# Products of 128 columns that nobody reads, in TensorE's waits at the start of a fused attention and expert kernel

## The chip, the cores and the metric

The kernel runs on one core of a Trainium2 chip. The metric is the device time of one execution in microseconds (us), as the median of several executions. The traced execution has a time of its own. Engines are named as the profile names them: PE is TensorE (matrix products and transposes), PEld is its weight load, DVE is VectorE, ACT is ScalarE, POOL is GpSimd, SP is the engine that issues most transfers.

## The reference

Three stages follow one another. First comes attention over 2 batches, 8 heads, 576 rows and 64 columns a head, in which each row of scores keeps only its 32 largest values:

```python
scores = scale * np.matmul(q, k.transpose(0, 1, 3, 2))
kth = np.partition(scores, -top_k, axis=-1)[..., -top_k:-top_k + 1]
scores = np.where(scores >= kth, scores, -1000000000.0)
attn = exp(scores - max) / sum
x = np.matmul(attn, v)
```

Then a top-1 mixture of 8 experts (512 to 1024 to 512 columns, 288 slots an expert), and last a dense layer (512 to 2048 to 512) with a rational function between its two products.

## The kernel before

**Tiling.** The 1152 rows of queries (both batches) are cut into 9 tiles of 128. A step of the attention is one tile and one head, so there are NH = 72 steps. `slot(i)` is what an engine does around step i; every engine has such a function, and all of them run through the same steps at different distances.

**What PE does in the attention.** Keys and queries are held as a high and a low part. `k_turn(g, half)` (line 1354) turns half a head of keys with six or three transposes of 96 columns and waits for the low part of that head, which DVE makes for heads 0 and 1 (line 766) and POOL for the others (line 605), out of what ACT made of the rows loaded (`k_high`, line 1110). `q_turn` (line 1367) turns four heads of queries, once for the high part and once for the low. ACT takes what was turned out of PSUM (`k_out`, line 1080, `q_out`, line 1101), but for the first high part of the queries, which DVE takes (line 775). `scores(x)` (lines 1389 and 1390) makes the 576 scores of a row in four products of 288 columns. It waits until keys and queries are turned and taken, and until DVE's first instruction on the scores before (`greater`, line 784) has freed the two banks `S_ps`. `turn_scores`, `less_max` and `drop` (lines 1401, 1411, 1418) turn the scores of step i - 2 into the other pair of banks, `T_ps`; nothing else is written there, and the first of them starts with slot 2. `times_v` (line 1435) multiplies by the values, from slot 3.

**What the others do.** ACT copies the scores to SBUF (`scores_out`, line 1123), POOL sums and subtracts the two halves of a row (lines 629 and 636), and DVE finds the 32 largest: line 784 once a step, then eight-wide maxima (lines 801 and 822) and replacements (lines 803 and 820). The smallest value kept goes to ACT for `short_of` (line 1131).

**The order at the start.** Each engine runs its program in order. PE's is: both halves of key head 0, queries high and low (heads 0 to 3), key head 1, `scores(0)`, `scores(1)`, key head 2, queries high and low (heads 4 to 7), key head 3, a wait for POOL's fill of the values' column of ones (`s_vo`, line 687), and then slots 0 to 71, where slot i begins with `scores(i + 2)` and slots 0 to 3 turn key heads 4 to 7. ACT's is: `k_high(0)`, `q_high(0)`, `k_high(1)`, `k_out` of head 0, `q_out` low, `k_out` of head 1, `k_high(2)`, `scores_out(0)`, `k_high(3)`, `scores_out(1)`, `k_out` of head 2, `q_out` high and low, `k_high(4)`, `k_out` of head 3, and then its slots, the first of which begins with `scores_out(2)`. Keys come in three transfers: heads 0 and 1, heads 2 to 7, and the second batch.

**The function used by the change.** `keep_busy` (line 1442) exists already; the kernel calls it between the experts and the dense layer with 512 columns:

```python
def keep_busy(times, to, by):
    for _ in range(times):
        nc.tensor.matmul(to, by[:, 0:P], by[:, 0:to.shape[1]], start=True, stop=True)
```

It signals nothing. `ones` is a constant of 128 by 128 that POOL writes first of all (line 594, after which `s_const` is 1).

Of the kernel before, what the change touches and what calls it, by code (L numbers as in the profile page):

```python
# [22 lines left out]
P = 128  # L23
# [5 lines left out]
NH = NT * H  # L29
# [28 lines left out]
def fused(nc, q, k, v, w_gate, w1, w2, w_in, w_out, a, b, out):  # L58

    ctx = ExitStack()  # L60
    with ctx:
# [5 lines left out]
        def sem(name):  # L67
            return ctx.enter_context(nc.semaphore(name))
# [81 lines left out]
        def small(name, shape, dt=F32):  # L150
            nonlocal o
            n = 2 if dt == BF16 else 4
            for d in shape[1:]:
                n *= d
            t = at(name, o, shape, dt)
            o += -(-n // 32) * 32
            assert base + o <= nc.sbuf_usable_end
            return t
        ident = small("ident", [P, P])
        tri = small("tri", [P, P], F32R)  # L160
        ones = small("ones", [P, P], F32R)
# [27 lines left out]
        T_ps = pb[1]  # L189
# [19 lines left out]
        s_const = sem("constants")  # L209
# [123 lines left out]
        def is_mixed(n):  # L333
            return n == MIXED

        def batches(n):
            return range(B) if is_mixed(n) else [n // (TPB + 1)]
# [6 lines left out]
        def k_pieces(i):  # L344

            n, h = divmod(i, H)
            if n == 0:
                return [(FIRST_K + h, half) for half in range(2)] if FIRST_K + h < H else []
            if n in (1, 2):
                return [(H + (n - 1) * (H // 2) + h // 2, h % 2)]  # L350
            return []
# [5 lines left out]
        def q_pieces(i):  # L357

            n, h = divmod(i, H)
            if h == 0:  # L360
                return [(n, 1, 1)] if 0 < n < NT else []
            if n >= LAST:
                return []
            return {3: [(n + 1, 0, 0)], 4: [(n + 1, 1, 0)], 7: [(n + 1, 0, 1)]}.get(h, [])

        def x_piece(i):

            n, h = divmod(i, H)
            return n - 1 if h == 6 and 0 < n < NT else None

        def logit_piece(i):

            n, h = divmod(i, H)
            if i == NH - 1:
                return LAST - 1
            return n - 2 if h == 0 and 1 < n < NT else None
# [27 lines left out]
        def emptied(use):  # L404

            assert use != BY_DVE
            return use + 1 - (use > BY_DVE)
# [928 lines left out]
        def _(pe):  # L1336
# [8 lines left out]
            def k_turn(g, half):  # L1345
                use = USE["k", g, half]
                if g < 2:
                    pe.wait_ge(s_kl[0], g + 1)
                else:
                    pe.wait_ge(s_kl[1], g - 1)  # L1350
                prep_in(use)
                for c in range(KJ // 2):
                    j = half * (KJ // 2) + c
                    last = nc.tensor.transpose(prep_bank(use)[:, c * KP:(c + 1) * KP],
                                               ks[g % KRING][:, j].rearrange("k t d -> k (t d)").bitcast(F32),
                                               ident[0:KP, 0:KP])
                last.then_inc(s_pf, 1)
# [12 lines left out]
            def scores(x):  # L1370

                n, h = divmod(x, H)
                if x == 0:
                    pe.wait_ge(s_pd, 1)
                pe.wait_ge(s_pe, max(emptied(USE["q", n, 1, h // (H // 2)]),
                                     max(emptied(USE["k", bb * H + h, 1]) for bb in batches(n))))
                if x:
                    pe.wait_ge(s_gr, x)
                for half in range(2):
                    dst = S_ps[:, half * BANK:half * BANK + HS]  # L1380
                    off = h * S + half * HS
                    if is_mixed(n):
                        for bb in range(B):
                            for low in range(2):
                                last = nc.tensor.matmul(dst, qTm[:, low, bb, h, :], kT[bb][:, off:off + HS],
                                                        start=(bb + low == 0), stop=(bb + low == 2))
                    else:
                        keys = kT[batches(n)[0]][:, off:off + HS]
                        nc.tensor.matmul(dst, qTh[:, h, :], keys, start=True, stop=False)
                        last = nc.tensor.matmul(dst, qTl[:, h, :], keys, start=False, stop=True)  # L1390
                last.then_inc(s_qk, 1)

            def turn_scores(x):

                pe.wait_ge(s_sc, x + 1)
                if x == NH - 1:
                    pe.wait_ge(s_gr, NH)
                elif x:
                    pe.wait_ge(s_ex, x)
                for j in range(KJ):  # L1400
                    nc.tensor.matmul(turned(x)[0:KP, j * P:(j + 1) * P], sc[x % NS][:, j * KP:(j + 1) * KP], ident[:],  # L1401
                                     start=(j in (0, 4)), stop=False, is_transpose=True, skip_group_check=True)

            def less_max(x):

                pe.wait_ge(s_mh, 2 * x + 2)
                for lo, hi in ((0, 4), (4, KJ)):
                    dst = turned(x)[0:KP, lo * P:hi * P].rearrange("k (j q) -> k j q", q=P)
                    each = minus_one[:].unsqueeze(1).to_broadcast([P, hi - lo, P])
                    for part in (mh, ml):  # L1410
                        nc.tensor.matmul(dst, part[x % 2][:].to_broadcast([P, KP]), each, start=False, stop=False,  # L1411
                                         skip_group_check=True)

            def drop(x):

                pe.wait_ge(s_so, x + 1)
                for j in range(KJ):
                    last = nc.tensor.matmul(turned(x)[0:KP, j * P:(j + 1) * P], so[x % 2][:, j * KP:(j + 1) * KP], minus_big[:],  # L1418
                                            start=False, stop=(j in (3, KJ - 1)), skip_group_check=True)
                last.then_inc(s_tt, 1)  # L1420

            def times_v(x):
                n, h = divmod(x, H)
                k_ = x // XG
                dst = bank(4 + k_ % 2)[:, (x % XG) * DV:(x % XG + 1) * DV]
                pe.wait_ge(s_ex, x + 1)
                if x < 2 * XG:
                    pe.wait_ge(s_pe, emptied(FIRST - 1))
                elif x % XG == 0:
                    pe.wait_ge(s_xe, k_ - 1)  # L1430
                for bb in batches(n):
                    pe.wait_ge(*((s_v[2], 16 * H) if bb else (s_v[1], 16 * (H - 2)) if h >= 2 else (s_v[0], 32)))
                    r_ = slice(bb * HALF, (bb + 1) * HALF) if is_mixed(n) else slice(0, P)
                    for j in range(KJ):
                        last = nc.tensor.matmul(dst[r_, :], pT[x % 2][:, j * P + r_.start:j * P + r_.stop],  # L1435
                                                vn[:, bb * H + h, j, :], start=(j == 0), stop=(j == KJ - 1))
                last.then_inc(s_pv, 1)
# [5 lines that stand above are left out]
# [57 lines left out]
                    last.then_inc(s_fx, 1)  # L1500

            def slot(i):
                if i + 2 < NH:
                    scores(i + 2)
                if 0 <= i - 3 < NH:
                    times_v(i - 3)
                if 0 <= i - 2 < NH:
                    turn_scores(i - 2)
                    less_max(i - 2)
                    drop(i - 2)  # L1510
                for k_ in k_pieces(i):
                    k_turn(*k_)
                for q_ in q_pieces(i):
                    q_turn(*q_)
                if x_piece(i) is not None:
                    turn_x(x_piece(i))
                if logit_piece(i) is not None:
                    logits(logit_piece(i))

            pe.wait_ge(s_ident, 3)  # L1520
            k_turn(0, 0)
            k_turn(0, 1)
# [2 lines left out]
            k_turn(1, 0)  # L1525
            k_turn(1, 1)
            scores(0)
            scores(1)
            k_turn(2, 0)
            k_turn(2, 1)  # L1530
# [3 lines left out]
            k_turn(3, 1)  # L1534
            pe.wait_ge(s_vo, 1)
            for i in range(NH):
                slot(i)
            for x in (NH - 2, NH - 1):
                turn_scores(x)
                less_max(x)  # L1540
                drop(x)
# [159 lines left out]
```

## Time and profile before

| what | value |
|---|---|
| time, median of 3 executions | 792.28 us (792.05 to 793.22) |
| time of the profiled execution | 790.87 us |
| its span, first to last instruction | 789.1 us |
| mean granted TensorE clock | 0.988 |
| PE busy | 750.9 us (95%), 5482 products |
| DVE busy | 664.5 us (84%) |
| ACT busy | 496.7 us (63%) |
| POOL busy | 368.5 us (47%) |

The span is the profiler's and leaves out 1.77 us that the execution's own time has around it. Busy times are sums over stages with different limits, so the share of an engine alone doesn't tell what sets the end. A product's duration includes its way through the array and overlaps with the next one, so the distance between two starts tells what a product costs. In a line of a timeline several alike are merged: the duration is then that of all of them.

### The profile page before, as it was taken

How to read it: one execution, taken by the hardware profiler on the slowest of the kernel's cores; microseconds unless marked ns; L12 is line 12 of the kernel's file. 1: busy time of each engine (PE TensorE's matmuls, PEld its weight loads, DVE VectorE, ACT ScalarE, POOL GpSimd, SP SyncE). 2: the span in 40 equal slices, each digit the busy share in tenths (PEclk: the TensorE clock that was granted, in tenths of full speed). 3: DMA queues.
4: the chain of work that ended last, by engine and by line, in shares of the span. 5: the costliest groups of instructions: out<-in, count | busy, mean ns of one | idle time of the engine just before them, and what ended most of it. 6: DMA issues, size and time to landing. Idle time of an engine off the chain costs nothing.

```text
span 789.1 us, 15796 instructions
## 1 busy us (share of the span) xinstructions
PE 750.9 (95%) x5482; PEld 700.7 (89%) x5482; DVE 664.5 (84%) x1677; ACT 496.7 (63%) x898; POOL 368.5 (47%) x540
## 2 busy tenths in 40 slices
PE   5899999999999999899999999999899999999997
PEld 4788899898888888789999999999779898998996
DVE  3999999999999999986666766675759998888885
ACT  6677777566677776474444444444547877677674
POOL 3746665554558785362000000000059778666764
PEclk8899999999999999999999999999999999999999
DMA  8640000800000203015475768686810002001001
GB/s 184 155 184 14 1 16 1 225 8 13 15 2 15 108 2 108 2 43 216 137 243 168 230 180 256 175 208 185 238 54 27 1 1 81 1 0 41 1 1 40
DMA packets 60811, 70.63 MB, mean 90 GB/s; under 512 B 21953, under 2 KB 40769, under 8 KB 60738
## 3 DMA queue, kind: packets, MB, share of 16 engines
q1 hardware_dynamic: 59298, 64.98, 28.6%
q0 software_dynamic: 1440, 4.72, 1.8%
q8 instruction: 41, 0.67, 0.4%
q14 instruction: 32, 0.26, 0.1%
HBM read 55.53 MB, written 14.16 MB: 88 GB/s over the span
## 4 chain that ended last, share of the span: by engine, by line
PE 58%; DVE 27%; DMA 5%; issue 5%; ACT 2%; POOL 2%; SPq 1%; DVEq 0%; ACTq 0%; POOLq 0%
PE bank L1564 16%; PE bank L1566 15%; PE bank L1565 15%; DVE best L801 9%; DVE pairs L803 6%; PE bank L1435 3%; DVE best L822 3%; DVE pairs L784 3%; DVE pairs L820 3%; DMA slots_out<-y_blocks 2%; PE bank L1411 2%; PE bank L1401 2%; DMA slot_rows<-slots_in 1%; DMA k_rows<-in_k 1%; DVE joined L831 1%
## 5 line engine op out<-in xcount | busy, mean ns | idle before, releaser
L1066 DVE RECIPROCAL r<-c 128x384 f32<-128x384 f32 x48 | 122.4, 2551 | 20.6 <-POOL c L740 19.7
L801 DVE MAX8 best<-pairs 128x8 f32<-128x288 f32 x288 | 116.8, 450 | 0.0
L1137 ACT ACTIVATE probsT<-bank 96x768 f32<-96x768 f32 x72 | 58.1, 807 | 90.8 <-PE bank L1418 88.4
L729 POOL DMA_INDIRECT x_rows<-slots_out,slot_index x9 | 10.5, 1165 | 210.2 <-DMA slots_out<-y_blocks 208.6
L1435 PE MATMUL bank<-v_rows,probsT 96*128 96x65 f32 (+1 forms) x960 | 105.8, 263 | 2.6 <-ACT probsT L1137 2.5
L1435 PEld LDWEIGHTS bank<-v_rows,probsT 96*128 96x128 f32 (+1 forms) x960 | 101.9, 181 | 6.8 <-ACT probsT L1137 5.6
L989 DVE TENSOR_TENSOR wl<-raw,wh 128x1024 fp32r<-128x1024 f32 x72 | 87.2, 1218 | 19.0 <-ACT wh L1245 18.9
L803 DVE MATCH_REPLACE8 pairs<-best,pairs 128x288 f32<-128x288 f32 x216 | 95.7, 450 | 0.0
L1262 ACT ACTIVATE hTh<-bank 128x288 fp32r<-128x288 f32 x64 | 26.4, 413 | 102.5 <-PE bank L1566 102.5
L629 POOL TENSOR_TENSOR pairs<-scores 128x288 int32<-128x288 int32 x72 | 57.5, 799 | 66.3 <-ACT scores L1123 66.0
L1245 ACT ACTIVATE wh<-raw 128x1024 fp32r<-128x1024 f32 x72 | 75.1, 1051 | 4.1 <-DMA raw<-in_moe_w_out 3.2
L1564 PE MATMUL bank<-xTh,wh 128*128 128x288 f32 x256 | 75.7, 296 | 1.0 <-DVE xTl L1006 0.7
L1564 PE MATMUL bank<-hTh,wh 128*128 128x288 f32 x256 | 75.7, 296 | 0.6 <-DVE hTl L1027 0.6
L1566 PE MATMUL bank<-hTh,wl 128*128 128x288 f32 x256 | 76.1, 297 | 0.0
L1565 PE MATMUL bank<-hTl,wh 128*128 128x288 f32 x256 | 75.8, 296 | 0.0
L1565 PE MATMUL bank<-xTl,wh 128*128 128x288 f32 x256 | 75.6, 295 | 0.0
L1566 PE MATMUL bank<-xTh,wl 128*128 128x288 f32 x256 | 75.1, 293 | 0.0
L740 POOL TENSOR_TENSOR c<-c,h 128x384 f32<-128x384 f32 x48 | 48.6, 1013 | 48.4 <-ACT h L1323 48.3
L1564 PE MATMUL bank<-x2h,wh 128*128 128x384 f32 x192 | 65.8, 343 | 0.5 <-DVE g L1073 0.3
L822 DVE MAX8 best<-pairs 128x8 f32<-128x288 f32 x144 | 66.1, 459 | 0.0
L1566 PE MATMUL bank<-x2h,wl 128*128 128x384 f32 x192 | 64.7, 337 | 0.0
L1565 PE MATMUL bank<-x2l,wh 128*128 128x384 f32 x192 | 64.4, 336 | 0.0
(160 smaller groups left out, 2195.5 us busy)
## 6 DMA issues: line engine op xcount, KB each, us to landing
raw<-in_moe_w SPq DMA_DIRECT2D x15, 2048.0 KB, 8.9
slots_in<-zeros SPq DMA_DIRECT2D x18, 256.0 KB
slots_out<-y_blocks SPq DMA_DIRECT2D x32, 144.0 KB, 8.1
raw<-in_moe_w_in SPq DMA_DIRECT2D x8, 512.0 KB, 8.0
slot_rows<-slots_in SPq DMA_DIRECT2D x28, 144.0 KB, 9.0
v_rows<-in_v SPq DMA_DIRECT2D x16, 144.0 KB, 4.2
out_rows<-out_rows SPq DMA_DIRECT2D x9, 256.0 KB, 2.4
q_rows<-in_q SPq DMA_DIRECT2D x8, 256.0 KB, 3.3
```

The costliest lines, as they stand in the source:

```text
L629: nc.gpsimd.tensor_tensor(pr[x % NPR][:, 1].bitcast(I32), of[:, 0:HS], of[:, HS:S], ALU.add).then_inc(s_ps, 1)
L801: ins = nc.vector.max(best, cur)
L803: ins = nc.vector.match_replace(cur, best, cur, NEG)
L822: ins = nc.vector.max(best, cur)
L989: nc.vector.tensor_tensor(piece(wl[slot], c), piece(raw[which], c), piece(wh[slot], c).bitcast(F32), ALU.subtract).then_inc(s_wl, 1)
L1066: nc.vector.reciprocal(rS[x][:], cS[x][:]).then_inc(s_d2, 1)
L1137: nc.scalar.activation(pT[x % 2][:], turned(x)[0:KP, 0:KJ * P], ACT.Exp, scale=SCALE).then_inc(s_ex, 1)
L1245: nc.scalar.activation(piece(wh[slot], c), piece(raw[which], c), ACT.Copy).then_inc(s_wh, 1)
L1435: last = nc.tensor.matmul(dst[r_, :], pT[x % 2][:, j * P + r_.start:j * P + r_.stop], vn[:, bb * H + h, j, :], start=(j == 0), stop=(j == ...
L1564: nc.tensor.matmul(dst, ah, bh, start=start, stop=False)
L1565: nc.tensor.matmul(dst, ah, bl, start=False, stop=False)
L1566: return nc.tensor.matmul(dst, al, bh, start=False, stop=stop)
```

## The change

Ahead of the first transposes PE waits for `ones` and multiplies `ones` by itself 40 times into the first 128 columns of `T_ps`. After `scores(0)` it does so 24 times. `scores(2)` and `scores(3)` are issued ahead of slots 0 and 1 rather than as their first piece (in the same place of PE's order), and after them stand 12 and 8 such products, and behind slots 0 and 1 another 6 and 14: 104 in all. The order of what was there stays, and nothing is changed on the other engines.

```diff
             def slot(i):
-                if i + 2 < NH:
+                if 2 <= i < NH - 2:
                     scores(i + 2)
...
+            pe.wait_ge(s_const, 1)
+            keep_busy(40, T_ps[:, 0:P], ones)
             pe.wait_ge(s_ident, 3)
             k_turn(0, 0)
...
             scores(0)
+            keep_busy(24, T_ps[:, 0:P], ones)
             scores(1)
...
             for i in range(NH):
+                if i < 2:
+                    scores(i + 2)
+                    keep_busy((12, 8)[i], T_ps[:, 0:P], ones)
                 slot(i)
+                if i < 2:
+                    keep_busy((6, 14)[i], T_ps[:, 0:P], ones)
```

## Rows read from the trace of the kernel before

**Rows 1.** Page, the span in 40 slices of 19.7 us: busy tenths and granted clock.

```profile
PE   5899999999999999899999999999899999999997
...
DVE  3999999999999999986666766675759998888885
...
PEclk8899999999999999999999999999999999999999
```

**Rows 2.** Stretches: length; busy us and (instructions) per engine; clock, DMA share, GB/s.

```profile
240.00:280.00 40.00, 37.16 (x322) 34.34 (x321) 40.00 (x157) 30.22 (x51) 31.42 (x52) 1.00 0.18 61
```

**Rows 3.** Timeline of VectorE: start us, us, what, count, [idle before it <- releaser].

```profile
14.94 0.46 DVE L784 TENSOR_TENSOR pairs<-bank,scores 128x288 f32<-128x288 f32 x1 [2.16 <-ACT scores L1123]
...
16.64 0.09 DVE L803 MATCH_VALUE_LOAD pairs<-best,pairs 128x8 f32 x1 [0.87 <-POOL pairs L636]
...
18.66 0.45 DVE L822 MAX8 best<-pairs 128x8 f32<-128x288 f32 x1
...
20.19 0.46 DVE L784 TENSOR_TENSOR pairs<-bank,scores 128x288 f32<-128x288 f32 x1 [1.09 <-ACT scores L1123]
...
24.79 0.44 DVE L784 TENSOR_TENSOR pairs<-bank,scores 128x288 f32<-128x288 f32 x1
```

**Rows 4.** Timeline of ScalarE, from 8 to 20 us.

```profile
8.27 1.19 ACT L1101 ACTIVATE qT_low<-bank 64x512 fp32r<-64x512 f32 x2 [1.29 <-PE bank L1367]
...
11.23 0.52 ACT L1110 ACTIVATE k_split<-k_rows 96x384 fp32r<-96x384 f32 x1 [1.04 <-DMA k_rows<-in_k]
...
14.26 0.65 ACT L1123 ACTIVATE scores<-bank 128x576 f32<-128x576 f32 x1 [1.56 <-PE bank L1390]
...
16.07 1.19 ACT L1101 ACTIVATE qT_high<-bank 64x512 fp32r<-64x512 f32 x2 [0.44 <-PE bank L1367]
...
18.51 0.52 ACT L1110 ACTIVATE k_split<-k_rows 96x384 fp32r<-96x384 f32 x1
...
19.52 0.64 ACT L1123 ACTIVATE scores<-bank 128x576 f32<-128x576 f32 x1
```

**Rows 5.** Timeline of TensorE's products, from 5 to 21 us.

```profile
5.33 1.19 PE L1354 MATMUL bank<-ident,k_split 96*128 96x96 f32 x6 [5.33 <-DVE k_split L766]
...
8.02 0.84 PE L1354 MATMUL bank<-ident,k_split 96*128 96x96 f32 x6
...
9.60 0.37 PE L1389 MATMUL bank<-kT,qT_high 128*128 128x288 f32 x1 [0.74 <-ACT qT_low L1101]
...
10.08 0.29 PE L1390 MATMUL bank<-kT,qT_low 128*128 128x288 f32 x1
...
12.93 0.58 PE L1389 MATMUL bank<-kT,qT_high 128*128 128x288 f32 x1 [2.56 <-DVE pairs L784]
...
13.78 0.44 PE L1390 MATMUL bank<-kT,qT_low 128*128 128x288 f32 x1
...
20.16 0.72 PE L1354 MATMUL bank<-ident,k_split 96*128 96x96 f32 x6 [1.34 <-POOL k_split L605]
```

**Rows 6.** Stretches of 1 us in which the granted clock changes; the column before DMA share.

```profile
11.00:12.00 1.00, 0.00 (x0) 0.00 (x0) 0.00 (x0) 0.77 (x2) 0.16 (x1) 0.90 0.81 153
...
18.00:19.00 1.00, 0.82 (x4) 0.51 (x3) 1.00 (x4) 0.97 (x3) 0.00 (x0) 0.69 1.10 244
...
22.00:23.00 1.00, 0.57 (x4) 0.57 (x5) 1.00 (x5) 1.00 (x3) 1.00 (x2) 0.52 1.15 188
```

**Rows 7.** Timeline of TensorE's products: eight short ones and what follows, full clock.

```profile
345.57 1.03 PE L1459 MATMUL bank<-wg,x_tileT 128*128 128x8 f32 x8 [0.17 <-issue]
...
346.46 0.77 PE L1495 MATMUL bank<-slot_of_token,x_high 128*128 128x288 f32 x4
```

**Rows 8.** Timeline of TensorE's weight loads at the lower clock.

```profile
17.49 0.33 PEld L1389 LDWEIGHTS bank<-kT,qT_high 128*128 128x128 f32 x1
...
17.70 0.33 PEld L1390 LDWEIGHTS bank<-kT,qT_low 128*128 128x128 f32 x1
```

**Rows 9.** Timeline of GpSimd: the constant that the new products read.

```profile
0.80 0.20 POOL L594 MEMSET ones<- 128x128 f32 x1 [0.29 <-POOLq L1690]
```

## The prediction

> **What bounds the kernel now.** I began with the page's slices. PE is busy at 9 tenths nearly everywhere, and the granted clock falls short in the first two slices alone, which is where the change works [rows 1]. DVE is at 9 in every slice from the third to the sixteenth. In a stretch of 40 us in the middle of the attention it is busy for all 40.00 us, PE for 37.16 [rows 2]. So the attention ends when DVE has done its list. A faster PE brings nothing there, unless it lets DVE begin its unbroken work earlier.
>
> Where does that begin? The timeline of DVE has its last long wait, 1.09 us for ACT's copy of the scores, ahead of the instruction at 20.19 [rows 3]. Whatever makes that copy earlier moves all that follows.
>
> So I followed ACT back [rows 4]. `scores_out(2)` at 19.52 comes behind a block without a pause that starts at 16.07. That block waited 0.44 us for PE's transposes of queries. The block before starts at 14.26, after 1.56 us of waiting for PE's `scores(1)`. Before that ACT waits for the second transfer of keys, which lands at 11.23: nothing that PE does can make that earlier.
>
> Last I read PE's clock. The windows show it fall to 0.50 within 11 to 12 us, rise in 18 to 19 and fall again at 22 [rows 6]. The value 1.00 at the very beginning is not to be believed: the six transposes take 1.19 us at 5.33, against 0.72 at 20.16, and 0.84 at 8.02 [rows 5]. So PE starts at the lower level, 1.2 GHz, and rises to 2.4 GHz near 8 us, some 2.7 us after its first product. `scores(0)` runs at full clock (9.60 to 10.08, 0.48 us from first to last start), `scores(1)` at half (12.93 to 13.78, 0.85 us) [rows 5]. In between PE waited 2.56 us for DVE, and the clock fell.
>
> **The price of one product.** None like it (128 columns, full weights) is in the trace. Eight products of 8 columns with weights as large take 0.89 us from 345.57 to 346.46 [rows 7], so 0.11 us each at full clock, a bound from weight loading. At half clock two loads start 0.21 us apart [rows 8]. Below, with streaming alone, it would be 0.85/3 x 128/288 = 0.126 us at half clock and 0.48/3 x 128/288 = 0.07 us at full [rows 5]. I take 0.11 and 0.21, since the loads are needed for each product; 0.07 and 0.126 are the lower ends.
>
> **40 ahead of the first transposes.** `ones` is written at 1.0 us [rows 9]; I start at 1.1. If the clock rises 2.7 us later as before, at 3.8, then 13 are done at 0.21 and 27 take 3.0 us: the end is at 6.8. If it rises only after 4.8 us, the end is at 7.2. The transposes were ready at 5.33 [rows 5], so PE starts them 1.5 to 1.9 us late. But they run at full clock by then. From 5.33 until ACT could take the low queries at 8.27 [rows 4] was 2.94 us; at twice the clock that is 1.5, so 8.3 to 8.7 instead of 8.27. ACT had 1.04 us to spare ahead of 11.23 [rows 4]. So this costs nothing; the cover ends if the first transposes start after 8.27 + 1.04 - 1.5 = 7.8 us.
>
> **24 after `scores(0)`.** The last of it starts at 10.08, so they run from about 10.2 (10.6 at the late end) for 24 x 0.11 = 2.64 us, to 12.8 (13.2). `scores(1)` began at 12.93 [rows 5]. Cost 0 to 0.3; I take 0.1 at most, since a later `scores(0)` is likely to be by less. What they buy: `scores(1)` at full clock. It is 0.37 us shorter from first to last start, and its last product shorter by 0.15 (0.44 against 0.29), so ACT's copy starts near 13.75 instead of 14.26: **0.5 us**.
>
> **Transposes between `scores(1)` and slot 0.** ACT got the queries' high part 1.81 us after it had got `scores(1)` (16.07 less 14.26), and had work for 1.37 of them [rows 4]. At twice the clock the 1.81 become 0.9, so the queries are there when ACT comes, and the 0.44 us of waiting go as well. ACT's list from 14.26 on then stands without a hole: 0.5 + 0.44 = 0.95 us earlier at `scores_out(2)`. `greater(2)` on DVE moves from 20.19 to 19.2 or 19.3. The next in line is DVE itself: its own last maximum of step 0, at 18.66 + 0.45 = 19.1 even if nothing before it moves [rows 3]. So not much more than 1.1 us can be had here.
>
> **12 after `scores(2)`, 6 after key head 4.** PE waited 1.34 us there for POOL's low keys [rows 5]; 12 x 0.11 = 1.3 fit in. The 6 put 0.66 us in front of `scores(3)`, which followed the transposes of 20.16 at once. It would come at 20.5 or so instead of 20.8. DVE wants `scores(3)` at 24.79 [rows 3], so it has more than 3 us in hand. Cost nothing.
>
> **8 after `scores(3)`, 14 after key head 5.** 22 x 0.11 = 2.4 us, between `scores(3)` (20.9 at the latest start before) and `scores(4)`, which cannot start before DVE's instruction of 24.79 [rows 3]: nearly 4 us, with one short transpose inside. Cost nothing. What they buy is that the clock doesn't fall at 22 us [rows 6]. `scores(4)` and the first turned scores run in half the time, but DVE had no hole after 20.19, so this is worth nothing at the end. No queue but PE's is passed: no transfer is added or moved, and nobody waits for the products.
>
> **Sum.** 0 for the 40, + 0 to 0.1 for the 24, - 0.5 and - 0.44 for ACT's list, 0 for the other 40 products: -0.95 us, between -0.85 and the -1.1 of DVE's own list. Against the profiled execution: 790.87 - 0.95 = 789.9. The runs' median is 1.41 above that execution; I carry the difference to it: 792.28 - 0.95 = 791.3 us. Everything after the attention follows in a chain, so the shift should last to the end. About 0.2% (1.6 us) is what a measurement can tell from none, and this is 0.12%.
>
> **The rivals.** (a) **The short products don't lift the clock** (slower). Half of a product's slot is weight loading, 0.11 against 0.05 of columns; in the trace the clock fell in spite of 1.4 us of work after 20.16 [rows 5, 6]. Then the 40 take 8.4 us and end at 9.5, later than the deciding point 7.8. The chain of 2.94 us at half clock follows, ACT gets the low queries at 12.4 instead of 8.27, 4.1 late less 1.04 of slack: +3.1. After `scores(0)` 24 x 0.21 = 5.0 us stand where PE waited 2.6: +2.4. Together +5.5, 797.8 us. At the lower end of 0.126 us the 40 end at 6.1 and are hidden, and the 24 cost 0.4: 792.7. Between the two ends, at 0.17, it is 1.1 + 6.8 + 2.94 - 8.27 - 1.04 = +1.5, and 4.1 - 2.6 = +1.5: 795.3. The likely half of it is 794.3 to 797.8. For it: no row shows the clock under such a mixture. Against: what was needed before 18.69 was no more than transposes and `scores(1)`.
>
> (b) **The transposes don't keep what the products won** (no change). The clock rises early but falls again over the transposes, and the 0.95 us are lost: 792.2. Against: the clock rose near 8 us when PE had done only transposes [rows 5], and in 18 to 19 us after mostly those [rows 6]. The Trainium skill ("TensorE: Matmul & The Clock Gate", Part 4) says that the full clock doesn't engage for transposes, since they don't count as busy in the same way; by that rule this rival would hold. The trace disagrees with it: 0.84 us for six transposes at 8.02 against 1.19 at 5.33.
>
> (c) **More than I see** (faster by 1.6 us and more): the runs stand 1.2 to 2.4 us above the profiled one, and if part of it is clock lost at the start, the products give that back too: 789.5 to 790.6. For it speaks only that difference.
>
> **How the numbers follow.** Forecast 0.55, (a) 0.20, (b) 0.12, (c) 0.13. Of the forecast a tenth or two reaches over 1.6 us by the measurement. Faster by over 0.2%: 0.13 + 0.10 = 0.23. Slower: 0.20, and 0.01 of mishaps. The rest, 0.56, within 0.2%. The range reaches down to 789.8, into (c), and up to 794.3, short of (a), which leaves out some 0.2 in all; the forecast's own range is 790.7 to 792.0.
>
> **What would show it.** Right: the first transposes start between 6.4 and 7.5 us with 0.72 us for six, products of line 1442 are 0.11 us apart, the clock reads 1.00 in every stretch up to 34 us, ACT's copy of `scores(1)` is at 13.7 and `greater(2)` at 19.2. The 24 end before DVE frees the banks. Wrong: products 0.21 us apart up to the end, transposes after 7.8 us, ACT's `k_high(2)` later than the transfer at 11.2, or a DVE wait that comes up after 20 us and takes the microsecond back.

## The result and the profile after

| | before | after |
|---|---|---|
| time, median | 791.90 us (788.66 to 793.22, 15 executions) | 797.61 us (794.36 to 801.88, 15 executions) |
| ratio | | 1.0085 (95% interval 1.0066 to 1.0105) |
| profiled execution, span | 790.87, 789.1 us | 797.61, 795.8 us |

The change made the kernel slower by 0.85%, and its executions spread wider. (The ratios in this document are estimates with an interval and not the quotient of the two medians, which is 1.0072 here. The two can differ by 0.1%, so effects of that size are read from traces.) I had forecast 791.3 us with a range of 789.8 to 794.3.

From the page of the changed kernel, its span and the slices that answer to [rows 1]:

```profile
span 795.8 us, 16004 instructions
...
PE   9999999999999999899999999999899999999997
...
DVE  1799999999999999986666667665759998888885
...
PEclk9999999999999999999999999999999999999999
```

The granted clock stands at 9 in all slices, where before it began with two eights. By this line the change did what it was for, and PE is full from the first slice. But DVE reads 1 and 7 where it read 3 and 9: it begins later. The 6.7 us that the span grew by all lie there. The last of DVE's searches (its smallest kept value of step 71) comes at 342.62 us, against 335.67 before, 6.95 later; `greater(2)`, the start of its unbroken work, comes 7.07 later.

PE's timeline of the changed kernel, as in [rows 5]:

```profile
1.06 8.80 PE L1442 MATMUL bank<-ones 128*128 128x128 f32 x40 [1.06 <-POOL ones L594]
...
9.65 1.18 PE L1354 MATMUL bank<-ident,k_split 96*128 96x96 f32 x6
...
13.91 0.58 PE L1389 MATMUL bank<-kT,qT_high 128*128 128x288 f32 x1 [0.41 <-ACT qT_low L1101]
...
14.77 0.45 PE L1390 MATMUL bank<-kT,qT_low 128*128 128x288 f32 x1
15.01 5.22 PE L1442 MATMUL bank<-ones 128*128 128x128 f32 x24
...
20.02 0.55 PE L1389 MATMUL bank<-kT,qT_high 128*128 128x288 f32 x1
...
25.25 0.41 PE L1389 MATMUL bank<-kT,qT_high 128*128 128x288 f32 x1
...
27.73 0.86 PE L1442 MATMUL bank<-ones 128*128 128x128 f32 x6
...
28.43 0.35 PE L1389 MATMUL bank<-kT,qT_high 128*128 128x288 f32 x1
```

The 40 products take from 1.06 to 9.65, **0.215 us each to the very end**, and the 24 take from 15.01 to 20.02, 0.209 us each. The clock doesn't rise in 8.6 us of unbroken products. `scores(0)` at 13.91 is slow as well (0.58 us for its first product; 0.37 at full clock, [rows 5]). It stays low to the last product of `scores(0)` (0.45 us at 14.77, 0.29 at full clock), so the transposes and `scores(0)` between 9.65 and 15.01 didn't lift it either in this execution. It rises near 25.3 us, when PE has done its transposes again and is in `scores(2)`; from there the same products take 0.12 us each (six from 27.73 to 28.43).

And this is how the window of 17 to 18 us reads in the middle of the 24 (columns as in [rows 2], the granted clock third from the end):

```profile
17.00:18.00 1.00, 1.00 (x7) 1.00 (x7) 0.00 (x0) 0.00 (x0) 0.73 (x1) 1.00 1.01 252
```

1.00, while every duration is at half clock. The record of the granted clock shows nothing before its first change. The clock line of the page was no witness here; the durations were.

ACT and DVE of the changed kernel, as in [rows 4] and [rows 3]:

```profile
12.58 1.19 ACT L1101 ACTIVATE qT_low<-bank 64x512 fp32r<-64x512 f32 x2 [1.30 <-PE bank L1367]
...
14.39 0.52 ACT L1110 ACTIVATE k_split<-k_rows 96x384 fp32r<-96x384 f32 x1
...
21.33 0.65 ACT L1123 ACTIVATE scores<-bank 128x576 f32<-128x576 f32 x1 [5.02 <-PE bank L1390]
```

```profile
15.93 0.46 DVE L784 TENSOR_TENSOR pairs<-bank,scores 128x288 f32<-128x288 f32 x1 [2.83 <-ACT scores L1123]
...
22.01 0.46 DVE L784 TENSOR_TENSOR pairs<-bank,scores 128x288 f32<-128x288 f32 x1 [5.62 <-ACT scores L1123]
...
27.26 0.46 DVE L784 TENSOR_TENSOR pairs<-bank,scores 128x288 f32<-128x288 f32 x1 [1.09 <-ACT scores L1123]
```

ACT gets the low queries 4.31 us late (12.58 for 8.27), starts `k_high(2)` 3.16 late (14.39 for 11.23) and the copy of `scores(0)` 3.59 late (15.25 for 11.66). DVE frees the banks at 16.39 (15.93 + 0.46), but PE is in its 24 products until 20.02: some 3.5 us more, since `scores(1)` follows the freeing by about 0.1 us. The wait that the 24 fill is only some 1.5 us long here (15.01 to about 16.5) and not 2.6: before, ACT made `k_high(2)` first and came to its copy of `scores(0)` late, and here it was ready for it. ACT's copy of `scores(1)` then comes 7.07 us late, and that accounts for the whole loss: 3.6 from the 40 and 3.5 from the 24.

### The profile page after: what moved, and what is told of

The parts are those of the page before. It is cut to its first block, busy times and chain, and to the rows that moved or that the text cites. A ratio compares the mean times of both kernels' runs of the same rounds, so it can differ in the third digit from the quotient of the medians.

```text
span 795.8 us, 16004 instructions
## 1 busy us (share of the span) xinstructions
PE 767.3 (96%) x5586; PEld 717.7 (90%) x5586; DVE 664.1 (83%) x1677; ACT 496.6 (62%) x898; POOL 369.4 (46%) x540
## 4 chain that ended last, share of the span: by engine, by line
PE 57%; DVE 26%; issue 5%; DMA 5%; ACT 3%; POOL 2%; SPq 1%; DVEq 0%; ACTq 0%; POOLq 0%
PE bank L1572 15%; PE bank L1573 15%; PE bank L1574 15%; DVE best L801 9%; DVE pairs L803 6%; PE bank L1435 3%; DMA slots_out<-y_blocks 3%; DVE best L822 3%; DVE pairs L784 3%; DVE pairs L820 3%; PE bank L1411 2%; PE bank L1401 2%; DMA slot_rows<-slots_in 1%; PE bank L1442 1%; DVE joined L831 1%
```

## The experiments

The theory after this: what lifts the clock is columns that stream through the array. A product of a 4-byte constant with 128 columns comes every 0.21 us at half clock. Its columns take half of that: 288 columns of `scores(0)` take 0.24 us (14.77 to 15.01), so 128 take 0.107. The rest goes to its weights, the array has a hole in each, and by this theory the clock stays low ("thin" below). Rivals: products of a constant don't count; short ones don't; nothing counts so soon after the start; the loss comes from the number of instructions alone.

**Each product wider.**

```diff
+            def wide_busy(times):
+                for _ in range(times):
+                    nc.tensor.matmul(T_ps[:, 0:4 * P].rearrange("p (j q) -> p j q", q=P), ones[:],
+                                     ones[:].unsqueeze(1).to_broadcast([P, 4, P]), start=True, stop=True)
-            keep_busy(40, T_ps[:, 0:P], ones)
+            wide_busy(10)
```

and 12, 6, 3, 4, 7 such products in the other places, in PE's order.

> The 104 products of 128 columns become 44 of 512 (10, 12, 6, 3, 4, 7), same weights, same constant, about the same time at each place as was planned. In the changed kernel a short product took 0.214 us while 128 columns stream in 0.107, so the array idled half of it for the weights. Theory 'thin': that half-idle stream doesn't lift the clock, full columns do. Then six transposes take 0.72 us at about 5.4, the clock reads full from about 4 us on, scores(1) takes 0.48 us from first to last start near 13, and the time is 0.95 us below before: ratio 0.9985 to 0.9995. Theory 'constant': products of ones alone don't lift it whatever their width. Then the 10 end near 5.4 at 0.43 us each, the 12 take 5.2 us instead of 2.6, and the time is 2.6 to 4 us above before: ratio 1.003 to 1.005. Theory 'early': PE can't rise so soon after the start; then the transposes are slow too at 5.4, but the 12 after scores(0) are fast.

Measured: 790.29 us, ratio 0.9996 (0.9980 to 1.0012). PE's timeline:

```profile
1.06 4.64 PE L1447 MATMUL bank<-ones 128*128 128x512 f32 x10 [1.06 <-POOL ones L594]
...
6.40 0.60 PE L1367 MATMUL bank<-ident,q_rows_high 128*64 128x128 f32 x4
...
12.17 0.30 PE L1389 MATMUL bank<-kT,qT_high 128*128 128x288 f32 x1
```

The same weights and the same ones now lift the clock: the queries are turned at full clock at 6.40 (0.60 us for four), and `scores(1)` starts at 12.17, at full clock. The first six transposes still took 1.05 us, so the rise came near 6 us and not near 4 as I had expected. "Constant" and "early" fall. From the landing of the keys, where ACT starts `k_high(2)` (10.20), to `greater(2)` (18.14) it is now 7.94 us, against 20.19 - 11.23 = 8.96 before: the start gains 1.02 us, as the forecast had it. The gain end to end can't be told from none.

**The first 40 taken away.**

```diff
-            pe.wait_ge(s_const, 1)
-            keep_busy(40, T_ps[:, 0:P], ones)
             pe.wait_ge(s_ident, 3)
```

> The changed kernel without its first 40 products; the other 64 stay. The trace of the changed kernel has 4.3 us of its loss at the 40 (first transposes at 9.65 instead of 5.33) and 2.9 at the 24 (5.0 us in place of a wait of 2.6). Theory 'thin': the transposes lift the clock near 8 us as before and scores(0) runs at full clock; the 24 then start at full clock (0.11 us each). If a thin stream can't even hold it, the clock falls near 12 us and the 24 end near 13.5: ratio 1.000 to 1.002. If it holds, the full gain of 0.95 us comes: ratio 0.9988. Rival 'all of it is the 40': ratio 0.9988 and nothing left. Rival 'the products after scores(0) cost as much whatever the clock': 2.9 us above before, ratio 1.0035.

Measured: 795.36 us, ratio 1.0060 (1.0039 to 1.0080), above all three expectations. PE's timeline:

```profile
5.63 1.19 PE L1354 MATMUL bank<-ident,k_split 96*128 96x96 f32 x6 [5.63 <-DVE k_split L766]
...
10.76 0.44 PE L1390 MATMUL bank<-kT,qT_low 128*128 128x288 f32 x1
11.00 5.22 PE L1442 MATMUL bank<-ones 128*128 128x128 f32 x24
...
18.03 0.88 PE L1367 MATMUL bank<-ident,q_rows_high 128*64 128x128 f32 x4
```

I had counted on a clock that rises near 8 us, as in the trace of before. In this execution it had not risen when the 24 came, 5.4 us after PE's first product, and it didn't rise in them: 5.0 us again, where a wait of some 1.5 us stood (DVE freed the banks at 12.38). It rose only in the transposes near 18.5, after they were over. So the 24 hurt by themselves. That they held the clock down is not shown by this run alone, for the 5.4 us of transposes and scores ahead of them hadn't lifted it either. What shows it best is the 40 of the changed kernel and of the next run: 8.6 us without a rise in both. The profiled execution is the third fastest of eight (793.2 to 797.8), so the slower ones lost more than this trace shows.

**Only the first 40.**

```diff
-            keep_busy(24, T_ps[:, 0:P], ones)
...
-                    keep_busy((12, 8)[i], T_ps[:, 0:P], ones)
...
-                    keep_busy((6, 14)[i], T_ps[:, 0:P], ones)
```

> Only the first 40 products; those after scores(0) to scores(3) and behind the slots are left out. Theory 'thin': first transposes at 9.65 at half clock, ACT's k_high(2) at 14.4 instead of 11.23, so everything 3.2 us late; the clock then rises in the transposes at 12 to 14 us and falls in the wait for DVE as before or not, +-1 us. Time 3 to 4 us above before: ratio 1.004 to 1.005. Together with the run without the 40 it should add up to the 1.0085 of the change. Rival 'the 40 are hidden behind the transfer of keys': ratio 1.000 and the whole loss in the 24.

Measured: 794.47 us, ratio 1.0049 (1.0030 to 1.0068), as expected: `k_high(2)` starts at 14.39, as in the full change. Alone the two parts cost 0.60% and 0.49%, together 0.85%. Both are there. I had expected them to add up to the 0.85%, and their sum is 1.09%. The intervals, each about 0.2% to either side, leave open whether that is more than noise. One thing differs: in this execution the clock is up by `scores(0)` at 13.91, in the changed kernel it isn't, after the same instructions.

**The same product, 2-byte.** The short ones once more, 128 columns in each, all ones, but 2-byte: on both sides of the product, weights and columns.

```diff
+        ones_bf = at("ones_bf16", o_raw, [P, P], BF16)
...
+            nc.gpsimd.memset(ones_bf[:], 1.0).then_inc(s_obf, 1)
             nc.gpsimd.memset(ones[:].bitcast(F32), 1.0).then_inc(s_const, 1)
...
+            def short_busy(times):
+                for _ in range(times):
+                    nc.tensor.matmul(T_ps[:, 0:P], ones_bf[:], ones_bf[:], start=True, stop=True)
...
+            pe.wait_ge(s_obf, 1)
+            short_busy(40)
```

and 24, 12, 8, 6, 14 in the places of the change.

> The same 104 products of 128 columns at the same places, but of a bf16 constant of ones instead of the 4-byte one (one more fill on GpSimd ahead of all, 0.1 to 0.2 us). In the trace of before bf16 products of 128 columns start 0.057 us apart at full clock, so the weight load hides and the columns stream without a hole. Theory 'thin' (what counts is the share of time in which columns stream): the clock rises within the 40, they end by about 4.5 us, transposes at 5.4 take 0.72 us for six, and the time is 0.5 to 0.95 us below before (the fills are shorter than planned, so the clock may fall in one of the waits): ratio 0.9985 to 1.000. Theory 'short products don't count' (their number of columns per instruction matters): the clock stays low, the 40 take 4.3 us at 0.107, end at 5.4, the 24 take 2.6 us: no delay and no gain, ratio 1.000 to 1.001, with transposes of 1.19 us at 5.4.

Measured: 790.07 us, ratio 0.9982 (0.9967 to 0.9998). PE, ACT's `k_high(2)` and DVE's `greater(2)` of this run:

```profile
1.06 3.84 PE L1450 MATMUL bank<-ones_bf 128*128 128x128 bf16 x40 [1.06 <-POOL ones_bf L596]
...
5.33 0.69 PE L1357 MATMUL bank<-ident,k_split 96*128 96x96 f32 x6 [0.43 <-DVE k_split L769]
...
9.02 1.51 PE L1450 MATMUL bank<-ones_bf 128*128 128x128 bf16 x24
...
12.12 0.37 PE L1392 MATMUL bank<-kT,qT_high 128*128 128x288 f32 x1 [1.59 <-DVE pairs L787]
```

```profile
10.43 0.52 ACT L1113 ACTIVATE k_split<-k_rows 96x384 fp32r<-96x384 f32 x1 [1.42 <-DMA k_rows<-in_k]
```

```profile
18.18 0.46 DVE L787 TENSOR_TENSOR pairs<-bank,scores 128x288 f32<-128x288 f32 x1 [0.34 <-ACT scores L1126]
```

40 products in 3.84 us, transposes on time at 5.33 and at full clock (0.69 us for six). Same number of instructions, same width, same constant: only the size of the numbers differs, and with it the distance between two products at full clock (24 end in 1.51 us, where the 4-byte ones take 2.8). 4-byte numbers by themselves aren't the reason either, since with 512 columns they lift the clock. What is left is a short product with a slow load of its weights, which is "thin". Seven traces of this document have these 40 2-byte products ahead of the transposes. In four the clock rose within them (3.72 to 4.00 us for all). In three they took 4.45 us, at half clock to the end, and the rise came right behind them or, at the latest, among the queries near 6.5 us: some 5.5 us after the first product, where 8.6 us of thin ones brought none. From the landing of the keys to `greater(2)` it is now 18.18 - 10.43 = 7.75 us, against 20.19 - 11.23 = 8.96 before: **1.21 us won at the start**.

**Lift with 2-byte products, hold with the 4-byte ones.** The first 40 as `short_busy`, the other 64 as in the change.

> The first 40 products are bf16, as in the run that was faster; the other 64 are the 4-byte products of the change. It separates lifting the clock from holding it. With bf16 the clock was full by the end of the 40 and scores(0) ran at full clock. Theory 'thin products neither lift nor hold': the 24 after scores(0) start 0.11 us apart and slow to 0.21 before their end, or the transposes after scores(1) are slow; scores(1) then starts 0.5 to 2 us late and the time is 0 to 2 us above before: ratio 1.000 to 1.003. Rival 'thin products cannot lift but can hold': the 24 take 2.7 us, end at 11.5 to 12, every row up to 25 us is at full clock, ratio 0.998 to 0.999 as with bf16 throughout.

Measured: 790.84 us, ratio 0.9994 (0.9976 to 1.0013). Its profiled execution, at 795.44 the slowest of its ten, shows why there is no simple answer:

```profile
9.12 2.79 PE L1445 MATMUL bank<-ones 128*128 128x128 f32 x24
...
12.05 0.37 PE L1392 MATMUL bank<-kT,qT_high 128*128 128x288 f32 x1
...
16.09 1.45 PE L1445 MATMUL bank<-ones 128*128 128x128 f32 x12
...
19.00 1.52 PE L1445 MATMUL bank<-ones 128*128 128x128 f32 x6
...
23.87 3.23 PE L1445 MATMUL bank<-ones 128*128 128x128 f32 x14
```

```profile
18.00:19.00 1.00, 0.93 (x7) 0.93 (x7) 0.90 (x3) 0.63 (x3) 1.00 (x6) 0.55 1.11 233
...
31.00:32.00 1.00, 1.00 (x11) 1.00 (x10) 1.00 (x4) 0.60 (x1) 0.51 (x4) 0.63 0.00 0
```

The 24 start at full clock and hold it (2.79 us), and so go `scores(1)` and the transposes. With the 12 and a wait of 0.52 us behind them the clock falls in 18 to 19 us, and from there to 31 to 32 us the thin products (0.21 us each again), two sets of scores and the turned ones don't bring it back. DVE waited 5.6 us in all after 20 us. In the profiles of the changed kernel and of the run without the 40 the same 12, 6, 8 and 14 held it, in the latter with a wait of 1.08 us behind the 12. So a thin stream can hold the clock, but not reliably. What decides between the two is not shown.

**Only the first 40, as 2-byte products.**

> Only the first 40 products, as bf16; PE's later waits stay empty. Theory 'the gain is in the later waits': the transposes at 5.3 and scores(0) run at full clock, which is worth nothing, since ACT waits for the transfer of keys until 10.2 to 11.2 all the same; the clock falls in the wait of 2.6 us for DVE, scores(1) is slow again (0.85 us from first to last start) and ACT's wait of 0.44 us is back. Ratio 1.000 within 0.001. Rival 'an early rise keeps the clock through the wait': scores(1) at 0.48 us, ratio 0.9985.

Measured: 790.67 us, ratio 1.0002 (0.9984 to 1.0020). The last product of `scores(0)` and the first of `scores(1)`:

```profile
8.83 0.29 PE L1393 MATMUL bank<-kT,qT_low 128*128 128x288 f32 x1
...
12.55 0.58 PE L1392 MATMUL bank<-kT,qT_high 128*128 128x288 f32 x1 [3.42 <-DVE pairs L787]
```

Full clock before the wait of 3.42 us, half after it; `greater(2)` is 8.97 us behind the keys, as before. So lifting the clock early is worth nothing by itself. It has to be kept until `scores(1)` starts.

**Only the later ones, as 2-byte products** (44, 22, 6, 12, 28, enough to fill the waits at 0.057 us each).

> No products ahead of the first transposes; the later ones as bf16, in numbers that fill the waits at 0.057 us each (44, 22, 6, 12, 28). Theory 'the gain is in the later waits': whether the clock rises in the transposes (5.3 to 9 us) or first in the 44, scores(1) runs at full clock or close to it; if the 44 start at half clock they take up to 4.7 us instead of 2.5 and delay scores(1) by up to 1 us. Ratio 0.998 to 1.001, wider spread from run to run than with the first 40. Rival 'without the 40 it is as slow as the 4-byte form without them' (1.006).

Measured: 792.83 us, ratio 1.0026 (1.0010 to 1.0042), above what I expected. The profiled execution, 1.5 us below that median, is not slow at the start: its clock rose just ahead of `scores(0)`, and the 44 took 2.63 us. Its clock fell at 29.8 us, after PE had waited 1.45 us behind slot 2, and DVE waited 1.5 us for it. The same wait of 1.45 us cost nothing in the first 2-byte run. Where the clock rises later the 44 would stand at half clock in the way. That may be why the median is worse, but no profile here caught it.

**All of it, with those larger numbers.**

> All in bf16 with the first 40 and the later numbers raised to fill the waits (44, 22, 6, 12, 28). Every row up to 25 us should be at full clock, as it already was with 24, 12, 6, 8, 14. Theory: VectorE's own list sets the beginning of its unbroken work, so more products buy nothing in the median: ratio 0.998 to 0.9995, greater(2) 7.7 to 8.0 us after the keys' transfer lands (9.0 in the trace of before). It may be steadier from run to run. Rival 'there is more in it': ratio under 0.997.

Measured: 790.93 us, ratio 1.0006 (0.9994 to 1.0019): no gain to be seen, though `greater(2)` was 7.75 us behind the keys as in the smaller form. That asked for another look at the later part. DVE's waits after 20 us, before and in the 2-byte form with 40 and 24 (us, times, longest):

```profile
DVE pairs L784 <- ACT scores L1123: 1.3, 2, 1.1
```

```profile
DVE pairs L787 <- ACT scores L1126: 1.6, 3, 1.0
```

Before, 1.09 of the 1.3 us is the one at 20.19 itself. The 2-byte form started its unbroken work earlier and then waited 1.6 us after all. PE and the windows at that place, and DVE's longest wait:

```profile
90.16 1.03 PE L1467 MATMUL bank<-wg,x_tileT 128*128 128x8 f32 x8 [0.59 <-ACT kT L1083]
...
91.66 1.58 PE L1438 MATMUL bank<-v_rows,probsT 96*128 96x65 f32 x12
...
93.03 1.49 PE L1404 MATMUL bank<-ident,scores 128*96 128x128 f32 x6
```

```profile
92.00:93.00 1.00, 1.00 (x10) 1.00 (x10) 1.00 (x7) 1.00 (x4) 0.00 (x0) 0.92 0.00 0
...
93.00:94.00 1.00, 1.00 (x7) 0.94 (x7) 1.00 (x5) 0.53 (x2) 0.91 (x1) 0.50 0.00 0
```

```profile
98.79 0.46 DVE L787 TENSOR_TENSOR pairs<-bank,scores 128x288 f32<-128x288 f32 x1 [0.95 <-ACT scores L1126]
```

At 90.16 PE has waited 0.59 us and does eight products of 8 columns for the gate's logits: weight loads with hardly a column between them. The clock falls at 92.9, after a set of scores and most of the products with the values, and `turn_scores` takes 1.49 us instead of 0.82. The larger form shows the same fall at the same place. My reading was that the kernel has a thin stretch of its own, which lowers the clock in some executions (three of the ten profiles up to then, in the third at 96.8 us, 2.5 us behind the start of the same eight products at 94.30). It isn't shown: the kernel before waits the same 0.59 us, does the same eight products in 1.03 us (at 92.25), and its clock stays full.

**Fills there too.** The 2-byte form (40, 24, 12, 6, 8, 14) with 24 products behind slot 2, where PE waits 1.45 us, and 10 ahead of the first logits:

```diff
                 if logit_piece(i) is not None:
+                    if logit_piece(i) == 0:
+                        for _ in range(10):
+                            nc.tensor.matmul(bank(4)[:, 3 * P:4 * P], ones_bf[:], ones_bf[:], start=True, stop=True)
                     logits(logit_piece(i))
...
+                if i == 2:
+                    for _ in range(24):
+                        nc.tensor.matmul(bank(4)[:, 3 * P:4 * P], ones_bf[:], ones_bf[:], start=True, stop=True)
```

> The bf16 form (40, 24, 12, 6, 8, 14) and two fills more: 24 such products behind slot 2, where PE waits 1.45 us for VectorE, and 10 ahead of the first gate logits, where it waits 0.59 us and then does eight products of 8 columns. In the profiles of the two bf16 runs with the first 40 the microsecond won at the start (greater(2) 7.75 us after the keys land, 8.96 before) was lost again: the clock fell at 92 us for 3.5 us, right behind those logits, and VectorE waited 1.6 us; in the bf16 run without the 40 it fell at 29.8 us. Theory 'the gain is real and given back by falls later': with the fills there is no fall in the attention, VectorE has no wait after 20 us, and the ratio is 0.997 to 0.999. Rival 'the clock falls there anyway' (the logits themselves are too thin): the fall at 92 us stays, ratio as with bf16 alone.

Measured: 789.12 us, ratio 0.9966 (0.9953 to 0.9978). DVE's waits from 20 to 338 us, and PE at the logits:

```profile
DVE pairs L787 <- ACT scores L1126: 0.2, 1, 0.2
...
DVE best_falling L948 <- DVE logits_less_max L946: 0.2, 1, 0.2
```

```profile
89.74 0.72 PE L1528 MATMUL bank<-ones_bf 128*128 128x128 bf16 x10
...
90.50 1.03 PE L1467 MATMUL bank<-wg,x_tileT 128*128 128x8 f32 x8
```

The wait of 0.59 us is filled, the clock is full through the rest of the attention, and DVE has two waits of 0.2 us left. Its last search comes at 333.89 us (335.67 before, 335.20 in the 2-byte form without these fills). Counted from the landing of the keys, which differs from execution to execution, that is 323.10 us, against 324.44 before and 324.77 in the 2-byte form: 1.3 us won.

> The bf16 form with the two further fills once more, unchanged, since its first result rests on 6 executions (0.9966, 0.9953 to 0.9978) and chance moves this kernel by 1.6 us at a time. Theory 'the start is worth 1 us and the falls avoided some more': ratio 0.996 to 0.9985, no wait of VectorE after 20 us but at most 0.2 us. Rival 'the first result was a lucky set': 0.999 to 1.000, as the bf16 form alone had it the second time.

The same kernel again: 789.65 us, ratio 0.9984 (0.9969 to 1.0000), last search at 333.69. By medians it is 1.7 and 1.0 us below before, and these are the two lowest medians of all that were run. The ratios, 0.9966 and 0.9984, stand beside 0.9982 and 0.9990 (below) for the 2-byte form without the two fills. Their intervals overlap.

**Only the fill at the logits**, in the kernel before.

> The kernel before with nothing but the 10 bf16 products ahead of the first gate logits. In its own profiled execution the clock did not fall there; in three of ten profiled executions of the variants it did, at a price of 1.6 us. Theory 'falls at the logits make part of the spread between executions': the upper end of the times comes down and the median by 0 to 0.8 us: ratio 0.999 to 1.000. Rival 'more products in PE's way cost': 10 x 0.057 us fit into the wait of 0.59 us, so at most 0.1 us, ratio 1.000 to 1.0005.

Measured: 790.98 us against 790.84, ratio 0.9989 (0.9979 to 0.9999). The medians say nothing and the ratio a little; I read no effect from it. In its profiled execution the clock fell elsewhere, at 20.2 us, and DVE waited 2.3 us after 20 us.

**The 2-byte form again.**

> The bf16 form of the change once more, unchanged, beside the same runs of before. It came out at 0.9982 (0.9967 to 0.9998), the form with more products at 1.0006 (0.9994 to 1.0019). Theory 'a gain of about 1 us that chance can hide': ratio 0.998 to 1.000. Rival 'no gain': 1.0000 or above.

Measured: 790.38 us, ratio 0.9990 (0.9977 to 1.0003). Its profile has no fall at the logits and its last search at 333.59, 323.16 behind the keys: with the 1.6 us kept, it looks like the form with all fills. (Its clock did fall for 3 us at 23.8, where no wait of DVE came of it.) So what the two fills add is not shown: a trace without them can be as good.

## Why the prediction was wrong

- **What bounds the start: right.** DVE's unbroken work begins with `greater(2)`, and what moves ACT's list moves the end: +7.07 us there became +6.7 in the span of the profiled execution.
- **The price of a product: right.** 0.21 at half clock and 0.11 at full were taken; 0.215 and 0.12 measured. The lower end of 0.126 us was too high: the first distance in `scores(1)` (0.37 us) is longer than the later ones (0.24 for 288 columns), and from those it is 0.107. The forecast didn't use it.
- **The step that failed** is "If the clock rises 2.7 us later as before, at 3.8, then 13 are done at 0.21 and 27 take 3.0 us". The row behind it showed transposes, and I carried their rise over to a product that I had priced myself, one paragraph earlier, as bound by its weight load. In the trace of before the transposes aren't bound by theirs:

```profile
14.02 1.16 PE L1354 MATMUL bank<-ident,k_split 96*128 96x96 f32 x6
14.98 1.06 PE L1367 MATMUL bank<-ident,q_rows_high 128*64 128x128 f32 x4
15.83 1.06 PE L1367 MATMUL bank<-ident,q_rows_low 128*64 128x128 f32 x4
```

  Those of keys come every 0.16 us (0.96/6) with 96 columns to stream, those of queries every 0.21 (0.85/4) with 128, though they have only half as many columns of weights. Those of keys have 128 columns of weights as well, and no 0.21 us goes by for them. The distance goes with the columns that stream, 1.7 ns for each at half clock, so nothing else holds a transpose up. Per us a transpose streams no more columns than the thin product (128 in 0.21). What sets the two apart is the pause in the thin one, and the runs with 512 columns and with 2-byte numbers, which have none, agree. The 40 ended at 9.65, past the deciding point of 7.8 that the text gives.
- **A second weakness of that step** is that it took one execution's rise as fixed. In the trace of before it came during the six transposes of 8.02, some 3 us after PE's first product. In the changed kernel and in the run without the 40 the same transposes and `scores(0)` ran for 5.4 us (9.65 to 15.01, 5.63 to 11.00) at half clock to the end.
- **The 24 after `scores(0)`** failed with the same step: 5.0 us for 2.64. They stood in a wait of some 1.5 us and not of 2.6, because `scores(0)` came late.
- **The rival that came true was (a)**, with both of its terms: +3.1 for the 40 (3.6 measured, as `scores(0)` ran slow too) and +2.4 for the 24 (3.5, for the shorter wait). That its total of 797.8 us meets the measured 797.6 is luck: in the profiled executions the loss is 7.07 us and not 5.5. The medians moved by 5.7 only, since the profiled execution of before stands 1.0 us below its median. I gave it 0.20 with "no row shows the clock under such a mixture". With its cause standing in rows 7 and 8 it deserved more than the forecast.
- **Rival (b)**, that transposes don't keep the clock, is refuted by the 2-byte form: there the clock is full through all transposes from 5.33 us on and in `scores(0)` behind them (0.37 us for its first product at 8.42). By the Trainium skill ("TensorE: Matmul & The Clock Gate", Part 4) transposes don't count as busy in the same way. The traces here disagree: the clock rose within transposes near 18.5 us without the 40, and in the trace of before with nothing but transposes done.
- **The gain of a held clock, forecast at 0.95 us,** is there in the 2-byte form: 1.21 us from the keys to `greater(2)`. ACT's copy of `scores(1)` comes 2.49 us behind the keys instead of 3.03 (0.54; 0.5 forecast), and the rest of ACT's list gives 0.67 (0.44 forecast).
- **"The clock reads 1.00 in every stretch up to 34 us" was a bad sign to name:** it came true in the run that was slow, for the record doesn't show a clock that is low from the start. I had seen that in the trace of before and didn't draw the conclusion.
- **Rival (c)** has something in it: executions of one kernel differ by when the clock rises and falls, and those with a higher mean granted clock are mostly the faster ones. But the products at the start don't cure that.

What stays open: why the changed kernel's times reach from 794.4 to 801.9. The moment of the rise differs between executions (between 8 and 9 us in the trace of before, after 11 in that without the 40), which may be it. The seven slowest (799.6 us and more) have a mean granted clock of 0.990 to 0.994, the eight others 0.991 to 0.997, so falls later on may have a part. Only one execution of the changed kernel was profiled. Open as well: what lowers the clock at 92.9 us in some executions, and whether the whole gain of about 1 us at the start reaches the end; the ratios of the 2-byte forms with all places filled lie from 0.34% below to 0.06% above before.

## What to carry to other kernels

Before using products to lift TensorE's clock, look whether their columns follow one another without a pause. Those that lifted it here did: 512 columns for each 4-byte load, or 128 with a 2-byte one. Those with a pause of half their time (128 columns, 4-byte) didn't in 8.6 us. Filling is worth it only where the slow stretch feeds the engine that sets the end, and a fill must be short enough to end before the wait does even at half clock. A gain won at one place can be given back by a fall of the clock elsewhere, so look through the whole bounding stage before calling it nothing.

## What the runs showed of the hardware that was not expected

- 40 products back to back for 8.6 us, at the lower of the two levels (1.2 GHz) from the first to the last; 40 of the same shape with 2-byte numbers were over in 3.84 us (4.45 in three other executions) with the clock at 2.4 GHz by the transposes behind them.
- The weight load follows the array's clock: short products with 4-byte weights of 128 columns come every 0.21 us at the lower level and every 0.11 to 0.12 at the upper, and with 2-byte numbers every 0.055 (44 from 10.21 to 12.65 us in the run without the first 40).
- A granted clock of 1.00 in the profile's windows can stand beside half-speed durations until the record's first change.
- PE can lose its clock with no long wait before: for 3.5 us at 92.9 us, with 0.59 us ahead of eight products of 8 columns as its only wait from 84 us on, and at 18.1 us behind a wait of 0.52. In other executions the clock stayed up over the same instructions.
- The moment at which the clock rises isn't fixed by the program: after the same instructions it was up at 13.91 us in the run with only the 40, and not in the changed kernel.
